# Gate products of the second layer taken from the experts' second weights, formed once inside the first sort, in a two-layer mixture-of-experts kernel

## The reference

```
h = f[:, t] * h + (1 - f[:, t]) * x[:, t]            # recurrence over the tokens
# first mixture: logits from normalised rows and expert_emb, divided by tau
out[mask] = gate_w * (relu(x[mask] @ w1[e]) @ w2[e])
# second mixture
logits = x @ w_gate                                  # x is the first one's output
expert_idx = argmax(logits, axis=1)
out[mask] = gate_w * (relu(x[mask] @ w1[e]) @ w2[e])
```

## Time and profile before

| | |
|---|---|
| median of 3 runs | 1380.84 us (1379.58 to 1381.11) |
| the profiled execution | 1380.53 us, of which the span in the trace is 1378.8 us |
| PE busy | 1326.5 us, 96% |
| DVE busy | 971.3 us, 70% |
| ACT busy | 836.0 us, 61% |
| mean granted clock of TensorE | 0.974 |

### The profile page before, as it was taken

One profiled execution on the slowest core, in us unless ns is written; L12 is line 12 of the kernel. 1 busy time (PEld: TensorE's weight loads), 2 busy tenths in 40 slices (PEclk: granted clock), 3 DMA queues, 4 the chain that ended last, 5 costly groups with the idle time before them and its releaser, 6 DMA issues.

```text
span 1378.8 us, 31340 instructions
## 1 busy us (share of the span) xinstructions
PE 1326.5 (96%) x11005; PEld 1296.1 (94%) x11005; DVE 971.3 (70%) x1468; ACT 836.0 (61%) x1402; POOL 440.5 (32%) x458
## 2 busy tenths in 40 slices
PE   7994799999999999999999999999999999999996
PEld 6892499999999999999999999899999999999996
DVE  5888476666666666679876679777777777777773
ACT  5774266666666666666656665556666666666663
POOL 4572222121121221222112144324444444444431
PEclk9995599999999999999999999999999999999998
DMA  7984686656665665668856657446666666666650
GB/s 275 327 273 93 90 260 198 202 199 193 217 198 191 210 199 195 199 204 142 262 157 201 212 194 229 162 154 221 221 217 213 222 224 217 224 214 217 223 185 1
DMA packets 189559, 276.83 MB, mean 201 GB/s; under 512 B 33351, under 2 KB 151765, under 8 KB 189493
## 3 DMA queue, kind: packets, MB, share of 16 engines
q1 hardware_dynamic: 175956, 240.74, 56.5%
q0 software_dynamic: 13536, 35.21, 7.7%
HBM read 242.69 MB, written 35.18 MB: 202 GB/s over the span
## 4 chain that ended last, share of the span: by engine, by line
PE 89%; DVE 6%; issue 2%; POOL 1%; ACT 1%; DMA 1%; SPq 0%; DVEq 0%; POOLq 0%; ACTq 0%
PE bank L1313 38%; PE bank L1331 37%; PE bank L1247 4%; PE bank L1297 3%; PE bank L1342 2%; PE bank L1351 1%; PE bank L1229 1%; PE bank L1210 1%; PE bank L1223 1%; DVE hT L389 1%; DVE gx L379 1%; DVE w1l L363 1%; POOL fg L894 1%; DVE hl L675 0%; DMA fin<-in_f_logit 0%
## 5 line engine op out<-in xcount | busy, mean ns | idle before, releaser
L1313 PE MATMUL bank<-xs,w1h 128*128 128x256 f32 x3008 | 570.3, 288 | 1.5 <-DVE xs L664 1.5
L1125 ACT ACTIVATE hh<-bank 128x512 fp32r<-128x512 f32 x376 | 225.3, 599 | 413.2 <-PE bank L1313 385.1
L1313 PEld LDWEIGHTS bank<-xs,w1h 128*128 128x128 f32 x3008 | 461.3, 189 | 3.2 <-DVE xs L664 1.9
L675 DVE SCALAR_TENSOR_TENSOR hl<-bank,hh 128x512 fp32r<-128x512 f32 x376 | 259.9, 691 | 249.3 <-ACT hh L1125 246.3
L1331 PE MATMUL bank<-w2h,hl 128*128 128x256 f32 x1504 | 423.1, 281 | 0.0
L1331 PE MATMUL bank<-w2l,hh 128*128 128x256 f32 x1504 | 422.4, 281 | 0.0
L1331 PE MATMUL bank<-w2h,hh 128*128 128x256 f32 x1504 | 421.7, 280 | 0.0
L1313 PE MATMUL bank<-xs,w1l 128*128 128x256 f32 x1504 | 421.5, 280 | 0.0
L1313 PEld LDWEIGHTS bank<-xs,w1l 128*128 128x128 f32 x1504 | 283.6, 189 | 0.0
L1331 PEld LDWEIGHTS bank<-w2h,hh 128*128 128x128 f32 x1504 | 283.3, 188 | 0.0
L1331 PEld LDWEIGHTS bank<-w2l,hh 128*128 128x128 f32 x1504 | 283.0, 188 | 0.0
(11 more groups left out here) (160 smaller groups left out, 1033.8 us busy)
## 6 DMA issues: line engine op xcount, KB each, us to landing
w1raw<-in_moe_w SPq DMA_DIRECT2D x94, 1024.0 KB
w2raw<-in_moe_w SPq DMA_DIRECT2D x94, 1024.0 KB, 5.5
rows_b<-yb SPq DMA_DIRECT2D x94, 128.0 KB, 2.1
xin<-in_x SPq DMA_DIRECT2D x19, 512.0 KB, 5.5
fin<-in_f_logit SPq DMA_DIRECT2D x19, 512.0 KB, 7.2
rows_a<-h_rows SPq DMA_DIRECT2D x19, 512.0 KB, 5.2
xb<-rows_a,row_i POOLq DMA_INDIRECT x94, 4.3
xb<-rows_b,row_i POOLq DMA_INDIRECT x94, 5.5
```

Source lines behind the costliest of these rows:

```text
L675: v.scalar_tensor_tensor(hl[:, j, :], bank[j % UB][:, :], 0.0, hh[:, j, :].bitcast(fp32), ALU.max, ALU.subtract).then_inc(hid_lo, 1)
L1125: nc.scalar.activation(hh[:, j, :], bank[j % UB][:, :], ACT.Relu).then_inc(hid_hi, 1)
L1313: ins = mm(bank[j % UB][:, f * GW:(f + 1) * GW], w[:, p, o:o + P], xs[:, p, a, c * GW:(c + 1) * GW], start=k == 0, stop=k == 3 * DC - 1)
```

## The change

The logits of the second gate are the outputs times `w_gate`, and the outputs are hidden rows times `w2[e]`. So `w2[e] @ w_gate`, 8 columns for each expert, can be formed once for the whole kernel, and put beside `w2[e]` as columns 256 to 263 of the down products.

- The 8 experts' second weights are loaded in 16 units of 512 KB (`load_unit`), 8 of them during the last chunks of the attention stage, into memory that other tiles use later.
- For each unit TensorE turns 8 blocks (`turn_w2`), ACT copies them in two pieces (`keep_turned`), and TensorE multiplies them as the moving operand (512 columns, float32) with a padded gate that stands still, 64 columns wide (`gate_w2`, 2 products, so 32 in all). These steps stand in PE's `routing()`: 3 ahead of the counting products, 4 behind them, one behind every third group of the table products, and the rest behind the last group.
- At the end the sums are copied, turned (`turn_gates`, 8 transposes of 64 columns) and copied again (`keep_gates`), and stored to memory, from which each pair of layer 0 loads its expert's 64 values per partition (`load_wg`); ACT and DVE split these too (`split_wg_hi`, `split_wg_lo`).
- The splits of pair 0's weights on ACT move from the start of the first sort to its last units.
- In layer 0 the down products have 264 columns in place of 256, and `turn_y`, `yT` and `y_logits` are gone. DVE keeps both tiles' logits with one copy from `yb`. Each output tile has a bank of its own.
- `resort(0)` and `resort(1)` start one step earlier, and count in 2 and 4 groups of experts (before: 2 and 2), in one bank.
- In pair 0, `down(0, 0)` comes behind `up(0, 3)`.

```diff
+            def turn_w2(u):
+                if u == 0:
+                    pe.wait_ge(rows_ok, NCH)
+                pe.wait_ge(all_in[u], 16)
+                for c in range(DC):
+                    wait(pe, w2t_ok, 2 * (u - 1) + c + 1)
+                    for n in range(FH):
+                        o = n * D + c * P
+                        ins = nc.tensor.transpose(bank[T_BANK[c]][:, n * P:(n + 1) * P],
+                                                  w2_units[u][:, o:o + P], ident[:, :])
+                    ins.then_inc(w2_turned, 1)
+            def gate_w2(u):
+                h, e = divmod(u, E)
+                pe.wait_ge(w2t_ok, 2 * u + 2)
...
+                for c in range(DC):
+                    o = (2 * (u % 2) + c) * 512
+                    ins = mm(bank[W_BANK[h]][0:GM, :], wg_pad[:, c, GM - E - e * E:2 * GM - E - e * E],
+                             w2_turn[:, o:o + 512], start=(e, c) == (0, 0), stop=(e, c) == (E - 1, DC - 1))
+                ins.then_inc(gate_ok, 1)
+            def gate_step(u):
+                if u < WUNITS:
+                    turn_w2(u)
+                if u > 0:
+                    gate_w2(u - 1)
...
             def routing():
                 T = TT
+                for u in range(EARLY):
+                    gate_step(u)
                 pe.wait_ge(dve_c, mark["oh"])
...
+                for u in range(EARLY, EARLY + SPREAD):
+                    gate_step(u)
+                u = EARLY + SPREAD
                 for q, t0 in enumerate(range(0, T, RC)):
-                    chunk(q, min(RC, T - t0), ST, 4, q == 0, t0 + RC >= T)
+                    chunk(q, min(RC, T - t0), ST, bank[TAB_BANK][:, 0:2 * ST], q == 0, t0 + RC >= T)
+                    if q % 3 == 2:
+                        gate_step(u)
+                        u += 1
+                for u in range(u, WUNITS + 1):
+                    gate_step(u)
+                turn_gates()
...
             def keep_turned(u):
+                wait(act, gate_ok, u - 1)
+                for c in range(DC):
+                    act.wait_ge(w2_turned, 2 * u + c + 1)
+                    o = (2 * (u % 2) + c) * 512
+                    nc.scalar.activation(w2_turn[:, o:o + 512], bank[T_BANK[c]][:, :],
+                                         ACT.Copy).then_inc(w2t_ok, 1)
...
-                            ins = mm(bank[Y_BANK + p][:, t * D:(t + 1) * D],
-                                     a[:, j, f * GW + t * P:f * GW + (t + 1) * P], w[:, p, o:o + D],
+                            ins = mm(bank[Y_BANK + rows_slot(i, t)][:, 0:n],
+                                     a[:, j, f * GW + t * P:f * GW + (t + 1) * P], w[p][:, 2 * j + f, 0:n],
```

More of the change, by code:

```diff
@@ L341, in _ @@
             mark["f"] = count[0]
+            link(v.tensor_copy(wg_pad[:, :, GM - E:GM], wg_T[:, :, :]))
+            mark["gate"] = count[0]
             link(v.reciprocal(rtau[:, :], tau_s[:, :]))
@@ L695, in _ @@
             m_x(Index(0))
+            split_wg_lo(Index(0))
             def step(i):
-                last, last2, nxt = i.plus(-1), i.plus(-2), i.plus(1)
-                if here(last2) and layer_of(last2) == 0:
-                    m_logits(last2, 0)
+                last, nxt = i.plus(-1), i.plus(1)
                 if here(i):
@@ L725, in step @@
                         split_w2_lo(nxt, 1)
+                    if here(nxt) and layer_of(nxt) == 0:
+                        split_wg_lo(nxt)
+                if here(last) and layer_of(last) == 0:
+                    m_logits(last)
                 tick(i, 3)
@@ L1175, in step @@
                         split_w2_hi(nxt, 0)
-                if here(last) and layer_of(last) == 0:
-                    m_yT(last, 0)
                 tick(i, 2)
@@ L1182, in step @@
                         split_w2_hi(nxt, 1)
+                    if here(nxt) and layer_of(nxt) == 0:
+                        split_wg_hi(nxt)
                 tick(i, 3)
@@ L1360, in step @@
             def step(i):
-                last, last2, nxt = i.plus(-1), i.plus(-2), i.plus(1)
+                last, nxt = i.plus(-1), i.plus(1)
+                first = i.var is None and i.const == 0
                 if here(i):
@@ L1379, in step @@
                     up(i, 2)
-                    down(i, 0)
-                if here(last) and layer_of(last) == 0:
-                    turn_y(last, 0)
+                    if not first:
+                        down(i, 0)
                 tick(i, 2)
@@ L1385, in step @@
                     up(i, 3)
+                    if first:
+                        down(i, 0)
                     down(i, 1)
-                if here(last) and layer_of(last) == 0:
-                    y_logits(last, 0)
                 tick(i, 3)
```

291 lines of the change are left out of this document (193 added, 98 removed).

## The result

The changed kernel takes 1356.73 us (median of 4, 1355.69 to 1357.01) against 1380.97 us for the kernel before on the same chip: a ratio of 0.9821, 95% interval 0.9809 to 0.9834. A later series of 5 gave 0.9812 (0.9799 to 0.9826). That is 24 us less, where 24 were forecast.

A forecast was written before the change was run, and what follows sets the result against it. PE, busy 96% of the span, was taken to bound the kernel. Against 1380.5 us, -61 (layer 0) + 7.5 (columns) + 28.4 (first sort) + 1 (waits) = -24 gave 1356 us, range 1343 to 1368.

The forecast's parts named there:

- Removed in layer 0: Layer 0's pairs: PE work taken out, 1.30 us a pair over 47 pairs, -61 us.
- Eight columns: Layer 0's down products: 8 more columns cost 3.3 ns a product, +7.5 us in all.
- Waits in layer 0: Layer 0: waits on ACT and DVE that the closer fit of shorter pairs can make, +1 us.
- Rival 4: Layer 0: DVE, ACT or late weights miss the shorter pair, 8 to 20 us given back, 1364 to 1376 us; chance 0.10.
- Price of a gate product: First sort: a float32 gate product of 512 columns costs 0.9 us, making a step 2.7 us at full clock.
- Rival 2: First sort: gate products cost the lower bound, 0.47 us each, a step 1.85 us; 1345 us; chance 0.12.
- The clock: First sort: PE's clock is full in dense gate steps and falls in each 8 us of table products.
- Rival 1: First sort: the clock holds through the table products, 8.6 us better, 1348 us; chance 0.20.
- Rival 3: First sort: the clock stays at half throughout, a step is 5.4 us, slower at 1392 us; chance 0.08.
- The walk: First sort followed stage by stage with the gate steps: pair 0's first product at 195.7 us instead of 166.28.
- The slow start of the first products: Pair 0's first 24 products: 1.9 us lost to the slow clock before, half of it given back, -1.0 us.
- Nothing waits: Transfers around the first sort: 8 MB more hold nothing up, and pair 1's weights have a whole pair to arrive.

The follow-up runs named there:

- experiment 1: Changed kernel without forming the gate products, the gates being a copy of other numbers, 264 columns kept: 1329.05 us, ratio 0.960 to the kernel before.
- experiment 2: Changed kernel with down products of 264 columns in layer 1 too, the additional columns unused: 1364.33 us, ratio 0.9859 to the kernel before.
- experiment 3: Changed kernel with half a gate step behind every group of 8 table products in the first sort, not a whole one behind every third: 1359.78 us.
- experiment 6: Changed kernel with the turned weights still and the gate moving, 8 products of 8 columns a unit, last transposes gone: 1381.37 us, ratio 0.9988.
- experiment 10: Changed kernel with all tile tables laid out tile by tile and a whole gate step behind every second table group: 1326.5 us, ratio 0.9595.
- experiment 4: Changed kernel with only `vals` laid out anew, the table products' moving columns side by side in memory: 1379.74 us, ratio 0.9968.

## Why the prediction was right

**Removed in layer 0 (-61).** Right. The pair is 11.94 us (11.95 forecast), and experiment 1 leaves 54 us once the gate steps are gone, forecast -61 + 7.5 = -53.5.

**Eight columns (+7.5).** Right: 3.3 ns a product in the chains of experiment 2, 7.5 us. The ratios there have 6.5, and the pairs' distance 8.8, of which 1.3 is not in the down products.

**Waits in layer 0 (+1).** About right. PE has one new wait there behind pair 0, 0.78 us at 607.9 us, where the first counting product of the second sort (line 1465) waits for DVE's `oh`. It is the only one until the end of layer 0. The window of PE, PEld and DVE that answers to the second of the earlier trace rows:

```profile
624.00:794.00 170.00, 170.00 (x1427) 169.72 (x1426) 134.30 (x223) 105.37 (x168) 43.19 (x45) 1.00 0.76 213
```

PE is never idle in it and DVE is at 79%, forecast 83. Rival 4 has its mechanism twice, in this wait and in pair 0 (below), but 2.3 us together and not 8 to 20: as a price it is out.

**Price of a gate product (0.9 us).** It is 1.86/2 = 0.93 us. Rival 2, the lower bound, is out. The estimate from the Trainium skill's four passes ("FP8 and Floating Point Precision", "TensorE Precision Notes") was 0.85, so the trace has 0.08 us more than that, and 0.03 more than the transposes' rate gave.

**The clock.** As forecast, it fell in the table phase, and the three steps there took 14.4 us against 14.7. Rival 1 is out. But part of the reason given was wrong. I used the attention stage, at 1.00 with transposes and 8-column products, against the Trainium skill's rule ("TensorE: Matmul & The Clock Gate", "Part 4 — PE-mode transpose") that transposes do not count as busy. In the sort the rule fits: turned units did not keep the clock up (experiment 3). Units with short products did not raise it in 110 us either (experiment 6), which the rule does not say, as these are no transposes. Rival 3 was nearer than its 8% say: with the other shape of the same products it is what happens.

**The walk.** Forecast and measured: counting 118.3 and 120.0, first tables 130 and 132.0, table phase over 171.6 and 173.7, last product 191.6 and 192.6, pair 0 195.7 and 196.0. That the end is met to 0.3 us is in part luck, for errors cancel. The counting came 1.7 us late, of which 1.0 is the slow start: the turns of the first two units and the products of the first took 3.84 and 2.93 us, 3.0 more than at full clock, where 2 were put in. The step is 2.88 us and not 2.7. Against that, the last part was given 2 us for a start at half clock, and the clock was back at 1.00 in the window from 172 us on; and the copies and turns at the end took 3.4 us instead of 4.1.

**The slow start of the first products (-1.0).** Mis-sized: the clock was full at 196 us, so all 1.9 us came back. This too has luck in it, since other kernels here with the same last steps enter pair 0 at half clock (experiment 10). And one step of the prediction failed, "Nothing waits" with "a whole pair to arrive" for pair 1's weights: they were asked for 1.55 us ahead of the first product, as forecast, but DVE needs them within pair 0, and PE waits 1.5 us. With the slow start of experiment 3 there is no such wait, so the two terms belong together, and what is left of the 1.9 us is 0.4.

Summed from pair 0 on: layer 0's pairs are 13.093 us before and 11.935 after, over four of them, and 47 x 1.158 gives -54.4. The seven pairs beside the second sort shrink by 6.5 us and not 8.1, +1.6, with the wait of 0.8 in it. The slow start gives -1.9, the wait in pair 0 +1.5, and layer 1 -1.8, since its pairs are 11.750 us instead of 11.788, again over four. That is -55.0, where the traces have -54.6; and +29.7 before it. The shorter pairs of layer 1 were not forecast. What makes them, perhaps the bank of its own for each tile, was not tested.

## What to carry to other kernels

A gain on the bounding engine can be read from the distance of its periods and held to a few per cent. What is put into its idle time elsewhere is free only as long as it is shorter than the gaps, and the first sort had some 24 us of gaps for 54 us of gate steps (16 x 2.88 = 46 at full clock). Where work on TensorE goes into a sparse stage, its shape decides its price twice, by its columns and by the clock that it brings about: the same sums with the other operand moving cost 26 us more. And where such a move makes one engine the bound of a stage alone, an old inefficiency of that engine that another one's time had nearly covered, here the strided tables, is worth twice as much to mend.

## What the runs showed of the hardware that was not expected

- A moving operand of 2-byte values 16 bytes apart costs TensorE about 1.8 ns a column at either clock: 0.341 us for 188 columns at 0.50 (26.94/79), and 0.231 us for 124 at 1.00 (1.85/8). Side by side 188 columns take 0.11 us at full clock and 0.18 at half (experiment 4).
- A DVE write of 752 2-byte values whose neighbours lie 376 bytes apart takes 3.4 us (experiment 4), with ACT writing to the same tile in the same way beside it, against 0.54 us side by side in the changed kernel. Which part the stride has and which the neighbour was not separated.
- TensorE can be busy in its records without a gap from 110 to 220 us and stay at the lower clock (experiment 6), when it runs transposes, 8-column products and strided table products.
- The attention stage, made of transposes and 8-column products, has 1.00 until 104 us in the kernel before and until 108 in the changed one. Why the clock holds there and does not rise in the sort of experiment 6 stays open; in both traces the record begins at 1.00.
